# Reordering the start of a fused attention and channel-mix kernel, and who squares in the last two chunks

## The reference

```python
scores = scale * q @ k.T            # window of 32 keys; heads 4 to 7: every 4th of 128
attn = exp(scores - max); attn = attn / (sum + 1e-9); x = attn @ v

x_prev = x shifted by one token, zero at each batch's start
xk = mu_k * x + (1 - mu_k) * x_prev
xr = mu_r * x + (1 - mu_r) * x_prev
k = max(xk @ w_k, 0)                # 512 -> 1024
x = sigmoid(xr @ w_r) * ((k * k) @ w_v)

h = x.T @ U @ V                     # token mix, rank 32
u = x + h.T
out = u + max(u @ w_ch1, 0) @ w_ch2 # 512 -> 2048 -> 512
```

## Time and profile before

| | before |
|---|---|
| median of 3 runs | 775.57 us (774.56, 775.57, 775.68) |
| the profiled execution, its own time | 774.65 us |
| its span, first to last instruction | 772.6 us |
| PE busy | 748.0 us, 97% of the span |
| DVE busy | 329.1 us, 43% |
| ACT busy | 296.1 us, 38% |
| POOL busy | 168.8 us, 22% |
| share of PE in the chain that ended last | 87% (DVE 7%) |

### The profile page before, as it was taken

How to read it: one execution, slowest core, us unless ns; L and a number is a source line. 1 busy time by engine, 2 the same in 40 slices (tenths; PEclk the granted TensorE clock), 3 DMA queues, 4 the chain that set the end, 5 groups by cost and what they waited for, 6 DMA issues and landing times.

```text
span 772.6 us, 13326 instructions
## 1 busy us (share of the span) xinstructions
PE 748.0 (97%) x5020; PEld 652.9 (85%) x5020; DVE 329.1 (43%) x696; ACT 296.1 (38%) x785; POOL 168.8 (22%) x257
## 2 busy tenths in 40 slices
PE   4799999999999999999999999999999999999998
PEld 3678888888888887788899989999999999999997
DVE  6788686768576747746311311311131131113111
ACT  4686767676777646534331111111111111112110
POOL 6897021202121133405871000000000000000000
PEclk9999999999999999999999999999999999999999
DMA  7874442333232101002430100100010000001001
GB/s 142 185 178 82 87 75 52 64 67 56 47 65 49 41 1 56 3 26 73 143 112 1 42 1 0 42 0 0 0 41 0 0 24 17 0 0 42 0 1 42
DMA packets 121747, 35.76 MB, mean 46 GB/s; under 512 B 109536, under 2 KB 115680, under 8 KB 121696
## 3 DMA queue, kind: packets, MB, share of 16 engines
q1 hardware_dynamic: 112000, 34.02, 18.1%
q10 hardware_dynamic: 9696, 1.05, 1.0%
HBM read 30.33 MB, written 4.72 MB: 45 GB/s over the span
## 4 chain that ended last, share of the span: by engine, by line
PE 87%; DVE 7%; issue 2%; ACT 1%; DMA 1%; SPq 1%; ACTq 0%; POOL 0%; DVEq 0%
PE bank L1242 26%; PE bank L1244 26%; PE bank L1243 26%; PE bank L1294 2%; PE bank L1283 2%; PE bank L1263 2%; PE bank L1323 1%; DVE xs_l L1079 1%; PE bank L1393 1%; DVE probs L1027 1%; DMA k_raw<-in_k_dram 1%; DVE sq_l L1089 1%; DVE sq L1085 1%; SPq L476 1%; DVE probs L1065 1%
## 5 line engine op out<-in xcount | busy, mean ns | idle before, releaser
L1212 DVE SCALAR_TENSOR_TENSOR h_l<-bank,h_h 128x384 fp32r<-128x384 f32 x96 | 53.5, 557 | 306.0 <-ACT h_h L966 306.0
L966 ACT ACTIVATE h_h<-bank 128x384 fp32r<-128x384 f32 x96 | 47.2, 491 | 326.1 <-PE bank L1244 326.1
L1242 PE MATMUL bank<-ut_h,w_h 128*128 128x384 f32 x384 | 130.5, 340 | 0.0
L1244 PE MATMUL bank<-ut_h,w_l 128*128 128x384 f32 x384 | 129.3, 337 | 0.0
L1243 PE MATMUL bank<-ut_l,w_h 128*128 128x384 f32 x384 | 128.8, 336 | 0.0
L1244 PE MATMUL bank<-w_h,h_l 128*128 128x512 f32 x288 | 113.7, 395 | 0.0
L1243 PE MATMUL bank<-w_l,h_h 128*128 128x512 f32 x288 | 113.5, 394 | 0.0
L1242 PE MATMUL bank<-w_h,h_h 128*128 128x512 f32 x288 | 112.0, 389 | 0.0
L1242 PE MATMUL bank<-xs_h,wk_h 128*128 128x256 f32 x288 | 85.7, 298 | 2.9 <-DVE xs_l L1079 2.0
L1243 PE MATMUL bank<-xs_l,wk_h 128*128 128x256 f32 x288 | 81.2, 282 | 0.0
L1244 PE MATMUL bank<-xs_h,wk_l 128*128 128x256 f32 x288 | 81.2, 282 | 0.0
(11 more groups left out here) (119 smaller groups left out, 1202.3 us busy)
## 6 DMA issues: line engine op xcount, KB each, us to landing
stage<-in_moe_w_ch_dram SPq DMA_DIRECT2D x16, 512.0 KB, 3.3
out_dram<-result SPq DMA_DIRECT2D x18, 256.0 KB, 2.1
q_raw<-in_q_dram SPq DMA_DIRECT2D x64, 40.0 KB, 2.1
q_raw<-in_q_dram SPq DMA_DIRECT2D x64, 32.0 KB, 2.1
v_raw<-in_v_dram SPq DMA_DIRECT2D x32, 64.0 KB, 2.3
k_raw<-in_k_dram SPq DMA_DIRECT2D x48, 40.0 KB, 2.1
k_raw<-in_k_dram SPq DMA_DIRECT2D x52, 32.0 KB, 2.0
stage<-in_moe_w_k_dram SPq DMA_DIRECT2D x3, 512.0 KB, 4.3
```

Source lines behind the costliest of these rows:

```text
L966: act.activation(h_h[:, m % KRING, :], h_bank[m % 2][:, 0:C2], ACT.Relu).then_inc(hh_done, 1)
L1212: dve.scalar_tensor_tensor(h_l[:, m % KRING, :], h_bank[m % 2][:, 0:C2], 0.0, h_h[:, m % KRING, :].bitcast(F32), op0=ALU.max, op1=ALU.subt ...
L1242: pe.matmul(dst, lhs[0], rhs[0], start=start, stop=False)
L1244: return pe.matmul(dst, lhs[1], rhs[0], start=False, stop=stop)
```

## The change

It has five parts. Line numbers of the changed file are 2 or 3 higher than those of the file before.

1. ACT issues the keys of pair 2 of part 1 right behind those of pair 1 and makes the shift of quarter 2, both ahead of its copy of C of pair 3 of part 0; before, the keys came four activations later, behind `high_first(3)`, and the shift came behind the copy.
2. DVE turns the first pair of part 1, A(1, 0), ahead of the copy D(0, 3) and of the last mixing, `mix(0, 3)`; `mix(0, 3)` comes ahead of `low_first(2)`. PE computes the scores B(1, 0) after 2 quarter units in place of 6. Later DVE turns A(1, 3) ahead of the copy D(1, 0) and of `square(0, 2)`.
3. In slot 6 of chunk 0 DVE normalises pair 3 of part 1 ahead of the slot's other steps, A(2, 1), B(2, 0) and D(1, 2), in place of after them.
4. In the last unit of each chunk DVE takes `xk`'s difference (`low_xk`) ahead of the normalisation, and in chunk 7 ahead of the token mix's step.
5. In chunks 7 and 8 ACT makes the full square, in place of DVE.

```diff
--- before
+++ changed
@@ -177,6 +177,8 @@
 
 
 MIX_CHUNK = NC1 - 2
+
+SCALAR_SQUARES = [0] + list(range(MIX_CHUNK, NC1))
 LATE = 2 * NUNIT
 
 
@@ -822,7 +824,7 @@
                 wait(act, unit_out, c * NUNIT + UNIT["k", m] + 1)
                 wait(act, v_mm, c * M1 + m - KRING + 1)
                 act.activation(sq_h[:, m % KRING, :], relu_k[:, m % 2, :], ACT.Square).then_inc(sqh_done, 1)
-                if c == 0:
+                if c in SCALAR_SQUARES:
                     act.activation(sq[:, m % 2, :], relu_k[:, m % 2, :], ACT.Square).then_inc(square_done, 1)
 
             def mix_step(kind, b):
@@ -920,8 +922,9 @@
             attention("C", 0, 2)
             first_shift(1)
             load_keys(1, 1)
+            load_keys(1, 2)
+            first_shift(2)
             attention("C", 0, 3)
-            first_shift(2)
             high_first(1)
             high_first(2)
             om_for_r(0, 0)
@@ -929,7 +932,6 @@
             mu_for_r(0, 0)
             om_for_r(0, 1)
             high_first(3)
-            load_keys(1, 2)
             mu_for_r(0, 1)
             shift_for_r(0, 2)
             shift_for_r(0, 3)
@@ -1080,7 +1082,7 @@
 
             def square(c, m):
 
-                if c > 0:
+                if c not in SCALAR_SQUARES:
                     wait(dve, unit_out, c * NUNIT + UNIT["k", m] + 1)
                     dve.tensor_tensor(sq[:, m % 2, :], relu_k[:, m % 2, :], relu_k[:, m % 2, :], ALU.mult)\
                         .then_inc(square_done, 1)
@@ -1132,22 +1134,23 @@
                     for t in range(KT):
                         if not last and n == MIX_SLOT[c][t]:
                             mix(c + 1, t)
-                    if c < MIX_CHUNK:
-                        for step in steps_in(slot + n):
-                            attention(*step)
-                        if n == NUNIT - 1:
-                            square(c, M1 - 1)
+                    soon = slot + n == FIRST_ONE["C"][3] - 1
+                    if soon:
+                        normalise(1, 3)
+                    for step in steps_in(slot + n) if c < MIX_CHUNK else []:
+                        attention(*step)
+                    if n == NUNIT - 1:
+                        square(c, M1 - 1)
+                        if not last:
+                            low_xk(c + 1)
+                    if c < MIX_CHUNK and not soon:
                         for k, p in normalised_in(slot + n):
                             normalise(k, p)
-                    else:
-                        if n == NUNIT - 1:
-                            square(c, M1 - 1)
+                    elif c >= MIX_CHUNK:
                         for step in mix_steps("vector", (c - MIX_CHUNK) * NUNIT + n):
                             mix_step(*step)
                 if last:
                     low_u(0)
-                else:
-                    low_xk(c + 1)
                 wait(dve, unit_out, c * NUNIT + UNIT["r", T1 - 1] + 1)
                 wait(dve, v_mm, (c + 1) * M1)
                 for t in range(T1):
@@ -1185,11 +1188,11 @@
             mix(0, 1)
             attention("D", 0, 2)
             mix(0, 2)
+            attention("A", 1, 0)
+            attention("D", 0, 3)
             low_first(1).then_inc(first_low, 1)
-            attention("D", 0, 3)
+            mix(0, 3)
             low_first(2).then_inc(first_low, 1)
-            mix(0, 3)
-            attention("A", 1, 0)
             low_first(3).then_inc(xkl_done, 1)
             attention("B", 1, 0)
             attention("A", 1, 1)
@@ -1200,9 +1203,9 @@
             square(0, 1)
             attention("B", 1, 2)
             normalise(1, 1)
+            attention("A", 1, 3)
             attention("D", 1, 0)
             square(0, 2)
-            attention("A", 1, 3)
             for c in range(NC1):
                 chunk(c)
 
@@ -1426,16 +1429,14 @@
                 attention(*step)
                 if step == ("C", 0, 3):
                     first_unit(0, 0)
-                elif step == ("D", 0, 3):
-                    first_unit(1, 0)
-                    first_unit(0, 1)
-                    first_unit(1, 1)
-                    first_unit(0, 2)
-                    first_unit(1, 2)
             for n in range(len(BEFORE)):
                 if TWO[n] < 2 and TWO[n] not in TWO[n + 1:]:
                     wait_drained(pe, GROUPS[n])
+            first_unit(1, 0)
             attention("B", 1, 0)
+            for t in range(1, KT - 1):
+                first_unit(0, t)
+                first_unit(1, t)
             first_unit(0, KT - 1).then_inc(unit_mm, 1)
             first_unit(1, KT - 1).then_inc(unit_mm, 1)
             unit(0, 2)
```

## The result

| | before | changed |
|---|---|---|
| median | 775.2 us (7 runs, 773.96 to 775.68) | 769.2 us (7 runs, 768.59 to 772.27) |
| ratio, 95% interval | | 0.9937, 0.9919 to 0.9956 |
| the profiled execution, its own time | 774.65 us | 768.66 us |
| its span | 772.6 us | 766.9 us |

A forecast was written before the change was run, and what follows sets the result against it. PE was taken as the bound, busy 748.0 of 772.6 us. 2.7 (chunks' ends) + 1.85 (chunk 7) + 0.8 (start) = 5.35 off 774.65 gave 769.3, plus 0.92 to the median: 770.2 us, range 768.4 to 773.6.

The forecast's parts named there:

- Chunks' ends: Ends of chunks 1 to 5: PE's five stalls for `xs_l` go, 2.7 us gained, bounds 2.0 and 3.1.
- the difference waits where it stands: Rival, chunks' ends: ACT's high part is late, normalisation held up, 2.7 shrinks to 0.5, 772.4 us; 4%.
- Chunk 7: PE's stalls for `sq_l`, `xs_l` and three shorter ones go: 1.85 us gained, bounds 1.0 and 2.4.
- the difference of about 1.15 us near 323.05: End of chunk 7: DVE's `xk` difference takes 1.15 us and ends near 323.05, 0.3 us before PE asks.
- ACT becomes the bound: Rival, chunk 7: ACT's 8 squares of 0.40 delay its other work, half of 1.85 stays, 771.3 us; 12%.
- The start: Chunk 0, parts 1 to 3: 0.1 + 0.6 + 0.2 = 0.9 us, 0.8 taken, bounds -1.0 and +1.7.
- The 0.65 at unit `k` 2: Start: unit `k` 2 begins at 32.1 in place of 32.79, 0.65 us gained, of which 0.1 is kept.
- Nothing in the change makes it sooner: Start, unit `r` 0: POOL's chain ends `xr` no sooner, `r` 0 stays near 41.7, PE waits.
- Slot 6: Chunk 0: the 1.22 us wait at 58.46 falls only in part; 0.2 us kept by B(2, 1).
- The transfers: Rival, start: earlier keys delay the weight piece, POOL 1.0 us late at `r` 0, 772.0 us; 13%.
- The clock: Rival, start: a gap in PE's matmuls keeps 1.2 GHz to 42 us, costing 18 us, 783 us; 3%.
- 0.55 each at either time: Start, argument against the transfers' collision: ACT's own four DMA issues took 0.55 us each at either time.

The follow-up runs named there:

- e2: The changed kernel with part 4 alone undone (the old order at the chunks' ends and in chunk 7): 772.49 us, ratio 0.9978.
- e3: The changed kernel with part 5 alone undone, so DVE makes the squares in chunks 7 and 8: 770.79 us, ratio 0.9964.
- e9: The kernel of e8 with unit 9 of chunk 7 squared by DVE again: 769.36 us, ratio 0.9932.
- e1: The changed kernel with parts 1, 2 and 3 undone, old order up to slot 6: 770.4 us, ratio 0.9943.
- e4: The changed kernel with only pair 2's keys issued at their old place, behind `high_first(3)`: 769.01 us, ratio 0.9928.
- e10: The edits of e9 and e4 together: 768.89 us, ratio 0.9931.
- e6: The changed kernel with part 3 alone undone, the normalisation of pair (1, 3) back behind slot 6's other steps: 769.25 us, ratio 0.9931.
- e8: The changed kernel with the edits of e5 and e7 together: 768.78 us, ratio 0.9924.
- c2: The changed kernel repeated without edit, beside e8, e9 and e10: median 770.58 us of five runs (770.86 with a sixth of 1048.2), ratio 0.9938.
- c1: The changed kernel repeated without edit, beside e1, e2 and e3: 768.88 us, ratio 0.993.
- e7: The changed kernel with B(2, 0) masked first in slot 6, then the normalisation, D(1, 2) and A(2, 1): 768.62 us, ratio 0.9937.
- e5: The changed kernel with A(1, 0) and the quarter units of part 2 in their old places on DVE and PE: 768.71 us, ratio 0.9926.

## Why the prediction was right, and which steps failed

The direction and the size were right, 5.35 us forecast against 5.7 in the span. For the chunks' ends and chunk 7 the mechanism was the one forecast; that the start's sum came out near is partly luck, as below. Step by step:

- **Chunks' ends: right.** 2.7 forecast, 2.99 gained, 3.01 when undone (e2). The 0.3 go with the short first matmul, which I had put only into the upper bound: at the end of chunk 1, 0.56 and 0.08 make the 0.64 measured. Reading the stall from the pitch, not from the row's 0.39, was needed: the view's sum as it stands gives 1.0 us too little. The rival *the difference waits where it stands* fell: no idle time ahead of 106.50.
- **Chunk 7: the place right, the size 0.3 too high.** The failed term is "the difference of about 1.15 us near 323.05". It took 1.60. With 1.22 it would have ended at 319.05, and PE asked at 319.32: the 0.3 us to spare were just there. By e3 nearly all of the gain is the squares'; by e2 part 4 adds 0.05. The rival *ACT becomes the bound* fell in its size: 1.55 of 1.85 came, not half, and e9 took ACT's last square away and chunk 7 grew. DVE's last `sq_l` does wait 0.71 us for ACT's square. That POOL's differences beside it slow DVE is what the traces point to, without an edit that tries it. Over the 14 profiled executions, 70 of the 112 differences ran with POOL idle, and each took 1.21 or 1.22; of the 42 with POOL at work beside them 28 took 1.59 to 1.76, and 14 took 1.20 to 1.22, that of e2 among them. So POOL's work is there in every long one, and doesn't make each one long. The Trainium skill has it in "GPSIMD Engine Reference", section "Specifications", that GpSimd shares its SBUF interfaces with VectorE, with contention for DVE instructions with two SBUF inputs. The square's 0.93 against 0.43 agrees; e2's 1.21 isn't explained by the sentence.
- **The start: 0.98 against 0.8, by other steps.** The 0.65 at unit `k` 2 came as worked out (32.14 against 32.1). The failed step is "Nothing in the change makes it sooner", and with it `r` 0 near 41.7, of which I kept 0.1: 0.73 us stayed, because POOL was 1.26 us sooner. This came with the transfers, not with the order of work: POOL began the mixing of `xr` 0.70 us sooner (32.29 against 32.99), after a piece of `w_r` that let it go on at 27.88 and not at 28.83, though SP had issued it later (23.22 against 22.46), and e1, with the old order, has the mixing at 32.25 as well. The rest is `w_v`'s piece, which SP issued at 31.24 and not at 32.63, behind its eight query issues. These took over 5.7 us in 6 of 14 profiled executions, with the keys late (the kernel before, e4, e10) and early (e3, e6, e8) alike. In four of the six `r` 0 began at 41.55 to 41.76, as forecast, in e10 at 41.08 and in e3 at 44.05; in seven of the eight others it began between 40.83 and 42.17, in c2 at 44.00. I had taken one execution's DMA timing for a property of the kernel. A(1, 3) gave 0.58 (0.6).
- **Slot 6: wrong in sign.** It gave -0.3 in place of 0.2: B(2, 0) to B(2, 1) grew from 4.66 to 4.98. 0.13 of this stands ahead of the transposes, which now wait for the masking behind the normalisation, a collision that the prediction named and priced too low; 0.19 stands behind them, where B(2, 1) comes 0.85 us after C(1, 3) and not 0.66, right after DVE's copy D(1, 2) has ended (58.08), which moved down as well and which the prediction didn't price. Where the keys of A(2, 1) land late, part 3 is needed all the same (e6); where they don't, PE took 3.83 us without it (e1).
- **What the start's edits are worth: not settled.** e1 against c1 says 0.3 us by chunk 1's start and 1.5 by the medians (of e1's six executions three have a lowered clock). e1's start is that of the kernel before, yet its chunk 1 began at 72.85 and not at 73.31: half of the 0.98 is in that difference and can't be put down to the change. Chunk 1 began at 72.33, 72.56 and 76.07 in three profiled executions of one program, so differences below 1 us there need more runs than these.
- **The transfers: fell, in another form.** The keys did not make POOL late: it ended `xr` between 40.40 and 41.46 with the keys early, e3 aside, and between 40.98 and 41.66 with them late. In e3 (43.05) POOL waited for `w_r` until 29.09 and then for ACT. The keys' issues were long once, in e3, at 2.6 us. By the Trainium skill's rule in "DMA: Bandwidth & Descriptors", section "Issuing engines are not separate DMA queues", the start's sum would have been the lower bound, -1.0; the times of POOL just given don't bear that out, and don't rule out that the transfers share engines.
- **The clock, 3%.** It did not decide the comparison, but a small form of it is real: in c2 and e6 the clock fell during the start, and in c2 it cost some 2.7 us (3.51 - 0.77). The kernel before has it too: 18 of its 45 executions in the three groups had a mean clock below 0.999, against 4 of 18 of the changed kernel, 3 of 6 of e1, 2 of 12 of e2, 3 of 12 of e3, 2 of 6 of e6 and of e7, 1 of 6 of e9, and none of the 20 of e4, e5, e8 and e10. It comes with either order at the start and with the keys early or late; no cause is shown.
- **Sums that don't come out.** The start's upper bound adds up to 0.9 + 0.55 = 1.45 by its own reason, not 1.7, which would put the lower end of the range at 768.6. The clock's rival, 18 us lost with 5.35 gained, is 788 us, not 783. And "0.55 each at either time" holds for ACT's four issues at 28 us; the four from 19.70 on took 0.33 to 0.49. None of these decides the result.

## What to carry to other kernels

Put the last piece that the next stage waits for ahead of work whose reader comes later, and check with the timeline how much later: here one change of order, at the ends of five chunks and without an added instruction, gave 3 of 6 us. Read a stall from the pitch of the matmuls, not from the wait noted on the row. And before resting a term on an idle time that a DMA or an issue ended, see whether it stands in a second execution; here the lengths of chunks 1 to 7 of one program repeated to 0.05 us, and the start, with its transfers, did not repeat to 3 us.

## What the runs showed of the hardware

- A VectorE instruction with two SBUF inputs varied by a factor of 2 in length, with nothing changed in the instruction: 0.37 to 0.96 us for the square of 128x256, 1.20 to 1.76 for the difference of 128x1024. With POOL idle beside it none of 436 squares took over 0.43 and none of 70 differences over 1.22. Over the changed kernel's eight differences, shortest, median and longest in ns:

```profile
L1081 DVE TENSOR_TENSOR xs_l<-xf,xs_h x8: 1212/1220/1605, 69.7 to 317.8; 128x1024 fp32r<-128x1024 f32 x8
```

- The length of DMA issues changed between executions: ACT's last keys ahead of the shift took some 0.5 us each in most executions and 1.2 in e3, and ACT's shift behind them came that much later (26.68 against 24.12 in c1).
- TensorE's granted clock fell to its lower level (1.2 GHz) at 39.5 us in one execution and not in another with nearly the same busy time from 36 to 39 us (1.43 and 1.40 of 3 us). In e6 it fell behind the 2.00 us wait at 58 us:

```profile
56.00:60.00 4.00, 2.00 (x26) 1.35 (x24) 3.90 (x7) 3.04 (x11) 3.92 (x6) 0.84 0.81 203
```
